# A mixed kernel of mLSTM and two expert layers: the recurrent state as one 40 by 41 block a head, and the scores of tile n beside the outputs of tile n - 1

## The chip, the cores and the metric

The kernel runs on one core of one Trainium2 chip. The metric is the device time of one execution in microseconds (us). Lower is better.

## What is computed

The reference has three stages, one behind the other (batch 2, 8 heads, 768 steps, head dimension 40):

```
for t in range(S):                       # mLSTM, for each batch and head
    m_new  = max(f[t] + m, i[t])
    C = exp(f[t] + m - m_new) * C + exp(i[t] - m_new) * outer(v[t], k[t])    # 40 x 40
    n = exp(f[t] + m - m_new) * n + exp(i[t] - m_new) * k[t]
    y[t] = sigmoid(o[t]) * (C @ q[t]) / max(|n . q[t]|, 1)
x = y as 1536 tokens x 320
x = (sigmoid(x @ w_gate) * (x @ w_val)) @ w_out            # layer one, d_ff 1536
x = rms_norm(x) * g;  a = x @ w_gate2
out = (a * sigmoid(a) * (x @ w_val2)) @ w_out2             # layer two
```

## The kernel before

**The recurrence.** It is cut into chunks of 128 steps. A tile n (0 to 11) is one chunk j = n // 2 of one batch b = n % 2, with all 8 heads. The state a batch carries from chunk to chunk is held as three groups of three heads: 120 partitions (3 heads by 40) and, a head, 41 columns (40 of v and a one for the normaliser). A product with k and v of three heads at once also gives blocks that mix heads, and a mask `bdm` takes these out.

The pieces of a tile are named by letters, and each engine has its own part of each:

- D: TensorE makes the logarithms of the decays of 8 heads in two banks (L936), ScalarE takes their exponential to `wexp` (L553) and copies the last column to `el` (L561); GpSimd multiplies v by it to `vk` (L469).
- S: TensorE makes the scores k q^T, two heads at a time in the two row halves of its array (L954, weights 40 x 128); VectorE multiplies them by `wexp` (L753); ScalarE takes the sigmoid of the output gate (L580).
- K: TensorE makes the tile's k^T v, three matmuls (L990); VectorE masks it by `bdm` (L792); GpSimd decays the state `cst` and adds the new part (L474, L477).
- N: TensorE makes state times q, three matmuls on 120 rows (L969), and scores times v, 16 matmuls whose outputs are halves of the array (L980); VectorE adds the two (L762, L764, L767).
- Y: VectorE's division: gate times numerator (L773), denominator and its reciprocal (L774, L775), their product to `y_tok` (L779), and a copy of its last 64 columns beside it (L781), because the third block of the transpose holds these columns twice.
- T: TensorE turns `y_tok` (three transposes, L895); ScalarE writes `x_hi` (L587), VectorE the rest `x_lo` (L808).
- R, F, A: decay factors of later chunks, their rows and their flattening DMA (L569, L575, L945, L946).
- O: the same turn as T for an output of layer one, for layer two (L895, L590, L812).

A matmul whose operands are plain fp32 (S, K, N) appears as two instructions in the trace, one of type fp32r as one.

**The layers.** Layer one takes the first 8 tiles in four blocks of two tiles (256 tokens). A block has 12 hidden units (`hidden`, 16 matmuls on 256 columns each, L1029 to L1032) and 4 halves of a projection (`project`, 18 matmuls on 320 columns each, L1096 to L1098). These are the 16 slots of a block. The last 4 tiles of layer one and all of layer two follow in four wide blocks of 512 tokens (`hidden_pair`, L1080).

**What sets the order.** Every engine runs its instructions in the order in which they are written. The table `WEAVE` says which pieces stand behind which slot; a slot is written "1.6" below (block 1, slot 6). All engines follow the same table:

```
for k in range(NB0):
    for slot in range(NF + 4):
        if slot < NF:
            gate(NF * k + slot)                  # VectorE: hf = sigmoid * value
        if 0 < slot <= NF:
            h_low(NF * k + slot - 1)             # VectorE: h_lo
        for what in WEAVE[k][slot]:
            piece(what)
```

On TensorE `gate` is the hidden unit itself; on ScalarE it is the unit's sigmoid (L626) and `h_high` (L632). T waits on TensorE until the whole of Y is done. The start is written out by hand: 24 idle matmuls (L1106), then D, S, N, K and T of tiles 0 and 1, D of tile 2 and R 1; then the first hidden unit, which waits for `x_lo` of both tiles and for two chunks of split weights. The split weights of layer one come from ScalarE (L538, L543) and GpSimd (L436, L441, L450), chunk after chunk during block 0 (`SPLIT_AT`); a hidden unit f waits for 2 (f // 3 + 1) chunks. Bank 7 is shared by N, R and O of the first six tiles; `seven` makes each of them wait for the one before (`IN_SEVEN`).

Of the kernel before, what the change touches and what calls it, by code (L numbers as in the profile page):

```python
# [4 lines left out]
F32 = mybir.dt.float32  # L5
# [14 lines left out]
GH = 3  # L20
NG = 3
KR = GH * D
KN = NG * KR
# [28 lines left out]

WEAVE = [
# [11 lines left out]
]  # L65

IN_SEVEN = [("R", 1)] + [what for block in WEAVE for slot in block for what in slot if what[0] in "NRO"]

# [3 lines left out]
def mlstm_moe_kernel(nc, gates, qk_t, q_t, vok, w_gv, w_o, rms_g, out):  # L72
# [5 lines left out]
    with ctx:  # L78
# [36 lines left out]
        QK, QT, VOK = 2 * NG * P + 2 * P, NG * P, HE + DM + KN  # L115

        with ExitStack() as late:
            def over(name, shape, dt):
                return late.enter_context(nc.sbuf_tensor(name, shape, dt))

            over("pad_step", [P, QK + QT + VOK], F32)
            more_lo = over("more_lo", [P, QK + QT + VOK], F32R)
            over("pad_rhs", [P, R, P], F32R)
            hf1 = over("hf1", [P, 2 * N1], F32)
        step = [sb(f"step{b}", [P, QK + QT + VOK], F32) for b in range(B)]
# [3 lines left out]
        cst = [sb(f"cst{b}", [KR, HE], F32) for b in range(B)]  # L129
        cnew = sb("cnew", [KR, HE], F32)  # L130
        inter = sb("inter", [P, HE], F32)
        num = sb("num", [P, HE], F32)
        bdm = sb("bdm", [KR, HE], F32)
# [4 lines left out]
        gcol = sb("gcol", [P, NJ, B, H], F32)  # L138
# [17 lines left out]
        q3 = [t[:, QK:QK + QT].rearrange("p (g t) -> p g t", t=P) for t in step]  # L156
        va = [t[:, QK + QT:QK + QT + HE] for t in step]
        o_sig = [t[:, QK + QT + HE:QK + QT + HE + DM] for t in step]
        kn = [t[:, QK + QT + HE + DM:QK + QT + VOK] for t in step]
# [34 lines left out]
        def kv_bank(n):  # L194
            return bank[(3, 1)[n]] if n < 2 else bank[4]
# [57 lines left out]
        q_in = [sem(f"q_in{b}") for b in range(B)]  # L253
# [61 lines left out]
        def _(sp):  # L315
            def load_qk(n):
                b = n % B
                if n >= B:
                    sp.wait_ge(s_done, 2 * (n - B) + 2)
# [3 lines left out]
            def load_vo(n):  # L323
# [4 lines left out]
                sp.dma_start(step[b][:, QK + QT:QK + QT + HE + DM], vok[n, :, 0:HE + DM]).then_inc(vo_in[b], 16)  # L328
# [47 lines left out]
            load_q(2)  # L376
# [4 lines left out]
            load_q(3)  # L381
# [809 lines left out]
```

## Time and profile before

| | us |
|---|---|
| median of 3 runs | 464.59 (464.55 to 464.93) |
| the profiled execution's own time | 464.66 |
| span of the profile, first to last instruction | 462.9 |
| TensorE busy | 452.5 (98%) |
| VectorE busy | 227.0 (49%) |
| ScalarE busy | 193.1 (42%) |
| GpSimd busy | 109.8 (24%) |
| mean granted TensorE clock | 0.996 |

The 1.8 us between span and time lie around the span. A busy TensorE is not yet one at its best: matmuls are pipelined, so the distance from start to start tells what one costs. 273 us of the span have passed when the first block of layer two begins.

### The profile page before, as it was taken

Reading aid. Unit: us, or ns where it says so; the run is one execution under the profiler, and the core shown is the slowest. Engines: PE = TensorE matmul, PEld = TensorE weight load, DVE = VectorE, ACT = ScalarE, POOL = GpSimd, SP = SyncE. Lnnn points to the kernel's source line nnn. Section 1 sums busy time; section 2 is a strip of 40 time slices with the busy share of each in tenths; the row PEclk is TensorE's granted clock in tenths of the full one; section 3 lists DMA queues with packets and bytes.
Section 4 is the critical chain, followed back from the end, with each engine's and each line's share of the span. In section 5 each row is a group of like instructions: output and inputs, shape, how many; then the busy total and the mean of one; then the engine's idle time right before and its main releaser. Section 6 shows DMA issues by size and latency. Waiting matters only on the chain. (4 is left out here: it accounts for less than half of the span.)

```text
span 462.9 us, 9428 instructions
## 1 busy us (share of the span) xinstructions
PE 452.5 (98%) x3923; PEld 410.1 (89%) x3923; DVE 227.0 (49%) x455; ACT 193.1 (42%) x359; POOL 109.8 (24%) x148
## 2 busy tenths in 40 slices
PE   8799999999999999999999999999999999999997
PEld 3699998999999999998888988889988889888897
DVE  8848866685556456432534226554026560056520
ACT  8877446642656463421745134322113321123310
POOL 5989910212121120000658354000000000000000
PEclk9999999999999999999999999999999999999999
DMA  7584610212221110300333200000000000000000
GB/s 255 193 274 134 203 53 30 68 50 83 76 62 46 61 45 5 150 1 2 99 107 95 87 19 25 1 1 16 28 16 1 1 0 30 30 0 1 2 28 30
DMA packets 11473, 27.89 MB, mean 60 GB/s; under 512 B 1526, under 2 KB 5830, under 8 KB 11430
## 3 DMA queue, kind: packets, MB, share of 16 engines
q1 hardware_dynamic: 11110, 27.20, 18.1%
q8 instruction: 31, 0.51, 0.5%
q10 hardware_dynamic: 320, 0.08, 0.1%
q14 instruction: 12, 0.10, 0.1%
HBM read 25.23 MB, written 1.97 MB: 59 GB/s over the span
## 5 line engine op out<-in xcount | busy, mean ns | idle before, releaser
L626 ACT ACTIVATE sg<-bank 128x256 f32<-128x256 f32 (+1 forms) x96 | 47.0, 491 | 147.4 <-PE bank L1080 101.1
L1080 PE MATMUL bank<-x_hi,wgv_hi 64*128 64x512 f32 x576 | 105.5, 388 | 0.8 <-DVE x_lo L812 0.8
L1080 PE MATMUL bank<-x_lo,wgv_hi 64*128 64x512 f32 x480 | 93.5, 386 | 0.0
L849 DVE TENSOR_TENSOR hf<-sg,bank 128x256 f32<-128x256 f32 (+1 forms) x96 | 53.1, 553 | 69.6 <-ACT sg L626 67.4
L1029 PE MATMUL bank<-x_hi,wgv_hi 128*128 128x256 f32 x288 | 81.9, 294 | 0.3 <-DVE x_lo L808 0.3
L1030 PE MATMUL bank<-x_lo,wgv_hi 128*128 128x256 f32 x288 | 79.4, 285 | 0.0
L1096 PE MATMUL bank<-wo_hi,h_hi 128*128 128x320 f32 x240 | 75.6, 315 | 0.0
L1080 PE MATMUL bank<-x_hi,wgv_lo 64*128 64x512 f32 x384 | 74.8, 386 | 0.0
L1098 PE MATMUL bank<-wo_hi,h_lo 128*128 128x320 f32 x240 | 74.2, 309 | 0.0
L1097 PE MATMUL bank<-wo_lo,h_hi 128*128 128x320 f32 x240 | 74.1, 309 | 0.0
L847 DVE TENSOR_TENSOR sg<-sg,bank 128x512 f32<-128x512 f32 x36 | 24.8, 688 | 87.3 <-ACT sg L626 85.3
L1080 PEld LDWEIGHTS bank<-x_hi,wgv_hi 64*128 64x128 f32 x576 | 53.9, 184 | 13.2 <-DVE x_lo L812 1.2
L1029 PEld LDWEIGHTS bank<-x_hi,wgv_hi 128*128 128x128 f32 x288 | 55.8, 194 | 1.5 <-DVE x_lo L808 0.4
L1030 PEld LDWEIGHTS bank<-x_lo,wgv_hi 128*128 128x128 f32 x288 | 55.9, 194 | 0.0
L1032 PE MATMUL bank<-x_hi,wgv_lo 128*128 128x256 f32 x192 | 54.8, 285 | 0.0
L1080 PEld LDWEIGHTS bank<-x_lo,wgv_hi 64*128 64x128 f32 x480 | 45.0, 184 | 9.3
L853 DVE TENSOR_TENSOR h_lo<-hf,h_hi 128x256 fp32r<-128x256 f32 (+1 forms) x84 | 50.4, 601 | 0.1
L1096 PEld LDWEIGHTS bank<-wo_hi,h_hi 128*128 128x128 f32 x240 | 45.1, 188 | 1.5 <-issue 1.1
L1097 PEld LDWEIGHTS bank<-wo_lo,h_hi 128*128 128x128 f32 x240 | 45.1, 188 | 0.0
L1098 PEld LDWEIGHTS bank<-wo_hi,h_lo 128*128 128x128 f32 x240 | 45.1, 188 | 0.0
L632 ACT ACTIVATE h_hi<-hf 128x256 fp32r<-128x256 f32 (+1 forms) x84 | 42.3, 504 | 5.7 <-DVE hf L849 5.7
L1080 PEld LDWEIGHTS bank<-x_hi,wgv_lo 64*128 64x128 f32 x384 | 36.0, 184 | 7.6
(131 smaller groups left out, 585.4 us busy)
## 6 DMA issues: line engine op xcount, KB each, us to landing
step<-in_vok SPq DMA_DIRECT2D x12, 324.0 KB, 2.9
step<-in_qk_t SPq DMA_DIRECT2D x24, 160.0 KB
step<-in_w_gv SPq DMA_DIRECT2D x6, 576.0 KB, 3.8
raw_p<-in_w_gv SPq DMA_DIRECT2D x5, 576.0 KB, 4.1
raw_x<-in_w_gv SPq DMA_DIRECT2D x5, 576.0 KB, 4.7
step<-in_vok SPq DMA_DIRECT2D x10, 180.0 KB, 3.4
step<-in_q_t SPq DMA_DIRECT2D x10, 180.0 KB, 2.8
raw_x<-in_w_o SPq DMA_DIRECT2D x3, 480.0 KB, 3.5
```

The source lines that it names most:

```text
L626: act.activation(sg_view(n), g_view(n), ACT.Sigmoid).then_inc(sg_done, 1)
L632: act.activation(h_view(n, 0), hf_view(n), ACT.Copy).then_inc(hhi_done, 1)
L847: dve.tensor_tensor(sg_view(n), sg_view(n), g_view(n), ALU.mult).then_inc(silu_done, 1)
L849: dve.tensor_tensor(hf_view(n), sg_view(n), v_view(n), ALU.mult).then_inc(hf_done, 1)
L853: dve.tensor_tensor(h_view(n, 1), hf_view(n), h_view(n, 0).bitcast(F32), ALU.subtract).then_inc(h_done, 1)
L1029: pe.matmul(ps, wgv_hi[:, wc, s, cs], x_hi[:, xs, s, :], start=(s == 0), stop=False)
L1030: mm = pe.matmul(ps, wgv_hi[:, wc, s, cs], x_lo[:, xs, s, :], start=False, stop=(s == 2))
L1032: pe.matmul(ps, wgv_lo[:, wc, s, cs], x_hi[:, xs, s, :], start=False, stop=False)
L1080: mm = pe.matmul(ps(n), w, x, start=own and (s, p) == (0, 0), stop=last and not own)
L1096: pe.matmul(ps, h_view(n0 + f, 0)[:, ts], wo_hi[:, f, :], start=(f == 0), stop=False)
L1097: pe.matmul(ps, h_view(n0 + f, 0)[:, ts], wo_lo[:, f, :], start=False, stop=False)
L1098: mm = pe.matmul(ps, h_view(n0 + f, 1)[:, ts], wo_hi[:, f, :], start=False, stop=(f == NF - 1))
```

## The change

The state of a head becomes a block of 40 by 41 of its own: the heads 0 to 3 lie on partitions 0 to 39 and the heads 4 to 7 on 64 to 103, each with four blocks of 41 columns. The mask, the padded groups of k and the separate copy of q (and its DMA) go. The product of state and q becomes a piece of its own, I: 16 matmuls of 40 x 64 weights, each in a quarter of the array, two outputs in each of two banks. S also becomes 16 matmuls of quarters (40 x 64) where it was 8 (40 x 128). K becomes 8 matmuls (128 x 40) in halves. The scores S of tile n stand in one slot with I, K and N of tile n - 1, the division Y one slot behind these, and the transpose T mostly one slot behind Y. VectorE's division multiplies the gate by the reciprocal first and then writes `y_tok` with two multiplications, one for the first 32 columns of each head (256), one for the last 8 twice (128); w_gate and w_val of layer one have their rows in the same order. At the start N and K of a tile stand together, and 10 idle matmuls stand between the pieces. In the first wide block VectorE's O stands ahead of `norm`, and ScalarE's last O ahead of its `square`.

```diff
 WEAVE = [
-    [[], [("S", 2)], [], [("K", 2), ("N", 2)], [("Y", 2)], [("D", 3)], [], [("S", 3), ("T", 2)],
-     [], [("K", 3), ("N", 3)], [("Y", 3)], [], [("A", 2, 0), ("A", 2, 1)],
+    [[], [("S", 2)], [], [("D", 3)], [], [], [("S", 3), ("I", 2), ("K", 2), ("N", 2)], [("Y", 2)],
+     [("T", 2)], [], [("I", 3), ("K", 3), ("N", 3)], [("Y", 3)], [("A", 2, 0), ("A", 2, 1)],
      [("A", 2, 2), ("T", 3), ("A", 2, 3), ("A", 2, 4)], [("F", 2)], [("R", 2)]],
-    [[("D", 4)], [("O", 0), ("A", 3, 0)], [("S", 4)], [("O", 1), ("A", 3, 1)], [("K", 4), ("N", 4)], [("Y", 4)],
-     [("D", 5)], [("T", 4), ("A", 3, 2)], [("S", 5), ("F", 3)], [("A", 3, 3), ("A", 3, 4)], [("K", 5), ("N", 5)],
-     [("Y", 5)], [("D", 6)], [("S", 6), ("T", 5)], [("K", 6), ("N", 6)], [("Y", 6)]],
-    [[("D", 7)], [("T", 6), ("O", 2), ("F", 4)], [("S", 7), ("O", 3)], [], [("K", 7), ("N", 7)], [("Y", 7)],
-     [("D", 8)], [("T", 7), ("R", 3)], [("S", 8)], [], [("K", 8), ("N", 8)], [("Y", 8)],
-     [("D", 9)], [("S", 9), ("T", 8), ("F", 5)], [("K", 9), ("N", 9)], [("Y", 9)]],
-    [[("D", 10)], [("T", 9), ("O", 4)], [("S", 10), ("O", 5)], [], [("N", 10)], [("Y", 10)], [("D", 11)], [("T", 10)],
-     [("S", 11)], [], [("N", 11)], [("Y", 11)], [], [("T", 11)], [], []],
+    [[("D", 4)], [("O", 0), ("A", 3, 0)], [("S", 4)], [("O", 1), ("A", 3, 1)], [("D", 5)], [("F", 3)],
+     [("S", 5), ("I", 4), ("K", 4), ("N", 4)], [("Y", 4), ("A", 3, 2)], [("T", 4), ("D", 6)], [("A", 3, 3), ("A", 3, 4)],
+     [], [("S", 6), ("I", 5), ("K", 5), ("N", 5)], [("Y", 5)], [("T", 5), ("D", 7)], [("F", 4)], []],
+    [[("S", 7), ("I", 6), ("K", 6), ("N", 6)], [("Y", 6)], [("T", 6), ("D", 8), ("O", 2)], [("R", 3)], [],
+     [("S", 8), ("I", 7), ("K", 7), ("N", 7)], [("Y", 7)], [("T", 7), ("D", 9), ("O", 3)], [("F", 5)], [],
+     [("S", 9), ("I", 8), ("K", 8), ("N", 8)], [("Y", 8)], [("T", 8), ("D", 10)], [], [],
+     [("S", 10), ("I", 9), ("K", 9), ("N", 9)]],
+    [[("Y", 9)], [("T", 9), ("D", 11), ("O", 4)], [("O", 5)], [], [("S", 11), ("I", 10), ("N", 10)], [("Y", 10)],
+     [("T", 10)], [], [("I", 11), ("N", 11)], [("Y", 11)], [("T", 11)], [], [], [], [], []],
 ]
...
+        def kv_view(n):
+            return bank[(3, 1)[n]][:, 0:KV] if n < B else bank[7][:, KV:2 * KV]
...
+        def state_view(i):
+            return bank[7][:, 0:KV] if i == 0 else bank[6][:, HE:HE + KV]
...
                 b = n % B
-                if n >= B:
+                if n >= 2 * B:
+                    sp.wait_ge(n_done, n - B + 1)
+                elif n >= B:
                     sp.wait_ge(s_done, 2 * (n - B) + 2)
...
             def divide(n):
                 b = n % B
                 src = num[:, :] if n >= B else bank[base(n) + 2][:, 0:HE]
                 dve.wait_ge(osig_done, n + 1)
-                link(dve.tensor_tensor(heads(o_sig[b]), heads(src)[:, :, 0:D], heads(o_sig[b]), ALU.mult))
                 link(dve.scalar_tensor_tensor(den[:, :], heads(src)[:, :, D], -1.0, den[:, :], ALU.mult, ALU.max))
                 link(dve.reciprocal(rden[:, :], den[:, :]))
+                link(dve.tensor_tensor(heads(o_sig[b]), heads(o_sig[b]), rden[:, :].unsqueeze(2).to_broadcast([P, H, D]),
+                                       ALU.mult))
                 if n >= B:
                     dve.wait_ge(t_done, n)
+
                 y = y_tok[:, y_slot(n), :]
-                link(dve.tensor_tensor(heads(y[:, 0:DM]), heads(o_sig[b]), rden[:, :].unsqueeze(2).to_broadcast([P, H, D]),
-                                       ALU.mult))
-                dve.tensor_copy(y[:, DM:3 * P], y[:, 2 * P:DM]).then_inc(y_done, 1)
+                dve.tensor_tensor(y[:, 0:2 * P].rearrange("p (h d) -> p h d", h=H), heads(src)[:, :, 0:Q],
+                                  heads(o_sig[b])[:, :, 0:Q], ALU.mult)
+                dve.tensor_tensor(y[:, 2 * P:3 * P].rearrange("p (u h d) -> p u h d", u=2, h=H),
+                                  heads(src)[:, :, Q:D].unsqueeze(1).to_broadcast([P, 2, H, D - Q]),
+                                  heads(o_sig[b])[:, :, Q:D].unsqueeze(1).to_broadcast([P, 2, H, D - Q]),
+                                  ALU.mult).then_inc(y_done, 1)
...
-                    for c in range(4):
-                        for i in range(2):
-                            rs = slice(64 * i, 64 * i + D)
-                            mm = pe.matmul(bank[base(n) + i][:, c * P:(c + 1) * P], sq[b][rs, 1, c, :], sq[b][rs, 0, c, :],
-                                           start=True, stop=True)
-                            if c == 3:
-                                mm.then_inc(s_done, 1)
+                    for c in range(HG):
+                        for u in range(2):
+                            us = slice(HALF * u, HALF * u + HALF)
+                            for i in range(2):
+                                rs = slice(HALF * i, HALF * i + D)
+                                mm = pe.matmul(bank[base(n) + i][us, c * P:(c + 1) * P], sq[b][rs, 1, c, us],
+                                               sq[b][rs, 0, c, :], start=True, stop=True)
+                                if c == HG - 1 and u == 1:
+                                    mm.then_inc(s_done, 1)
+                elif kind == "I":
+                    if j == 1:
+                        pe.wait_ge(cn_done, b + 1)
+                    else:
+                        pe.wait_ge(cst_done, n - 2 * B + 1)
+                    pe.wait_ge(r_exp, part_of(j))
+                    seven(what)
+
+                    pe.wait_ge(x_done, n)
+                    for c in range(HG):
+                        cs = slice(c * D1, (c + 1) * D1)
+                        for u in range(2):
+                            us = slice(HALF * u, HALF * u + HALF)
+                            for i in range(2):
+                                rs = slice(HALF * i, HALF * i + D)
+                                pe.matmul(state_view(i)[us, cs], sq[b][rs, 0, c, us], cst[b][rs, cs], start=True, stop=True)
...
+                    for c in range(HG):
+                        for i in range(2):
+                            h = HG * i + c
+                            mm = pe.matmul(kv_view(n)[HALF * i:HALF * i + D, c * D1:(c + 1) * D1], kn[b][:, h * D:(h + 1) * D],
+                                           vk[b][:, h * D1:(h + 1) * D1], start=True, stop=True)
...
-            for _ in range(24):
-                pe.matmul(bank[6][:, :], zeros[:, 0:P], zeros, start=True, stop=True)
-            for kind in "DSNKT":
+
+            def idle(ps, count):
+                for _ in range(count):
+                    pe.matmul(ps[:, :], zeros[:, 0:P], zeros, start=True, stop=True)
+
+            idle(bank[6], 23)
+            idle(bank[3], 1)
+            for kind in "DS":
                 for n in range(B):
                     piece((kind, n))
+            idle(bank[7], 4)
+            for n in range(B):
+                piece(("N", n))
+                piece(("K", n))
+            idle(bank[7], 4)
+            piece(("T", 0))
             piece(("D", 2))
+            idle(bank[7], 2)
+            piece(("T", 1))
             piece(("R", 1))
```

## Rows read from the trace of the kernel before

**Rows 1.** The page, busy time of TensorE: us, share, instructions.

```profile
PE 452.5 (98%) x3923; PEld 410.1 (89%) x3923; DVE 227.0 (49%) x455; ACT 193.1 (42%) x359; POOL 109.8 (24%) x148
```

**Rows 2.** Waits of TensorE: us in total, times, longest.

```profile
PE bank L895 <- DVE x_lo L812: 1.0, 2, 0.7
...
PE bank L1080 <- DVE x_lo L812: 0.8, 1, 0.8
PE bank L969 <- DVE x_lo L812: 0.7, 1, 0.7
...
PE bank L990 <- DVE tail L753: 0.3, 1, 0.3
```

**Rows 3.** Timeline of TensorE, score piece of a tile: start, us, instruction.

```profile
89.93 0.28 PE L1030 MATMUL bank<-x_lo,wgv_hi 128*128 128x256 f32 x1
90.14 1.16 PE L954 MATMUL bank<-step 40*128 40x128 f32 x16
...
91.46 0.28 PE L1030 MATMUL bank<-x_lo,wgv_hi 128*128 128x256 f32 x1
```

**Rows 4.** Timeline of TensorE, pieces K and N of a tile.

```profile
95.05 0.28 PE L1030 MATMUL bank<-x_lo,wgv_hi 128*128 128x256 f32 x1
95.18 0.76 PE L990 MATMUL bank<-tail,step 128*120 128x123 f32 x6
95.78 0.83 PE L969 MATMUL bank<-cst,step 120*128 120x123 f32 x6
96.54 1.13 PE L980 MATMUL bank<-step,tail 128*64 128x41 f32 x32
...
97.83 0.28 PE L1030 MATMUL bank<-x_lo,wgv_hi 128*128 128x256 f32 x1
```

**Rows 5.** Timeline around a division, block 1: TensorE, ScalarE, VectorE.

```profile
99.50 0.28 PE L1030 MATMUL bank<-x_lo,wgv_hi 128*128 128x256 f32 x1
...
99.82 0.38 ACT L626 ACTIVATE sg<-bank 128x256 f32<-128x256 f32 x1 [3.75 <-PE bank L1030]
...
100.91 0.48 DVE L773 TENSOR_TENSOR step<-num,step 128x320 f32<-128x320 f32 x1
...
102.40 0.20 DVE L781 COPY y_tok<-y_tok 128x64 f32<-128x64 f32 x1
```

**Rows 6.** VectorE from 28 to 58 us by shape: busy, mean ns.

```profile
L853 DVE TENSOR_TENSOR h_lo<-hf,h_hi 128x256 fp32r<-128x256 f32 x10 | 8.4, 835 | 0.0
...
L779 DVE TENSOR_TENSOR y_tok<-step,rden 128x320 f32<-128x320 f32 x2 | 2.0, 1023 | 0.1
```

**Rows 7.** Timeline of GpSimd at the start: splits of weight chunks.

```profile
19.91 1.00 POOL L441 TENSOR_TENSOR wgv_hi<-raw_x,wgv_hi 64x384 fp32r<-64x384 f32 x1
...
34.56 1.00 POOL L441 TENSOR_TENSOR wgv_hi<-raw_x,wgv_hi 64x384 fp32r<-64x384 f32 x1
```

**Rows 8.** Timeline of ScalarE, the exponentials of a tile.

```profile
69.60 1.28 ACT L553 ACT_TABLE_LOAD   x1
70.90 1.09 ACT L553 ACTIVATE tail<-bank 128x512 f32<-128x512 f32 x2
72.08 0.22 ACT L561 ACTIVATE el<-tail 128x8 f32<-128x8 f32 x1
```

**Rows 9.** Timeline of TensorE at the start.

```profile
19.93 0.55 PE L895 MATMUL bank<-ident,y_tok 128*128 128x128 f32 x3 [1.79 <-DVE y_tok L781]
...
21.66 0.58 PE L1029 MATMUL bank<-x_hi,wgv_hi 128*128 128x256 f32 x1 [0.31 <-DVE x_lo L808]
```

**Rows 10.** Stretches: us, busy us (count) of five engines, PEclk, DMA share, GB/s.

```profile
21.80:24.90 3.10, 3.10 (x15) 3.10 (x16) 0.61 (x2) 3.00 (x7) 2.15 (x3) 0.50 0.92 327
```

**Rows 11.** The page, DMA issues: count, KB each, median us to landing.

```profile
step<-in_vok SPq DMA_DIRECT2D x12, 324.0 KB, 2.9
```

**Rows 12.** Timeline before layer two: ScalarE's and VectorE's last O.

```profile
271.94 0.48 ACT L590 ACTIVATE x_hi<-bank 128x384 fp32r<-128x384 f32 x1
...
273.64 0.55 DVE L812 TENSOR_TENSOR x_lo<-bank,x_hi 128x384 fp32r<-128x384 f32 x1
```

More of the change, by code:

```diff
@@ L53, with mlstm_moe_kernel @@
 WEAVE = [
[2 rows of a table removed]
[2 rows of a table added]
      [("A", 2, 2), ("T", 3), ("A", 2, 3), ("A", 2, 4)], [("F", 2)], [("R", 2)]],
[8 rows of a table removed]
[9 rows of a table added]
 ]
-IN_SEVEN = [("R", 1)] + [what for block in WEAVE for slot in block for what in slot if what[0] in "NRO"]
+IN_SEVEN = [("R", 1)] + [what for block in WEAVE for slot in block for what in slot if what[0] in "IRO"]
 SPLIT_AT = {0: [4], 2: [5], 3: [6], 4: [7], 5: [8], 7: [9], 8: [10], 9: [11]}
-def mlstm_moe_kernel(nc, gates, qk_t, q_t, vok, w_gv, w_o, rms_g, out):
+def mlstm_moe_kernel(nc, gates, qk_t, vok, w_gv, w_o, rms_g, out):
     ctx = ExitStack()
@@ L119, in over @@
                 return late.enter_context(nc.sbuf_tensor(name, shape, dt))
-            over("pad_step", [P, QK + QT + VOK], F32)
-            more_lo = over("more_lo", [P, QK + QT + VOK], F32R)
+            over("pad_step", [P, STEP], F32)
+            more_lo = over("more_lo", [P, STEP], F32R)
             over("pad_rhs", [P, R, P], F32R)
             hf1 = over("hf1", [P, 2 * N1], F32)
-        step = [sb(f"step{b}", [P, QK + QT + VOK], F32) for b in range(B)]
+        step = [sb(f"step{b}", [P, STEP], F32) for b in range(B)]
         d_rhs = sb("d_rhs", [P, R, P], F32R)
@@ L128, in mlstm_moe_kernel @@
         l_row = sb("l_row", [2 * Q, LR * P], F32R)
-        cst = [sb(f"cst{b}", [KR, HE], F32) for b in range(B)]
-        cnew = sb("cnew", [KR, HE], F32)
+        cst = [sb(f"cst{b}", [KR, KV], F32) for b in range(B)]
+        cnew = sb("cnew", [KR, KV], F32)
         inter = sb("inter", [P, HE], F32)
         num = sb("num", [P, HE], F32)
-        bdm = sb("bdm", [KR, HE], F32)
         ones = sb("ones", [R, P], F32)
@@ L665, in _ @@
                     m = M0 + T1 * k + t
-                    if k == 0:
+                    if k == 0 and t < T1 - 1:
                         square(m)
                         piece(("O", M0 - B + t))
+                        continue
+                    if k == 0:
+                        piece(("O", M0 - B + t))
+                        square(m)
                         continue
@@ L883, in _ @@
                     for t in range(T1):
+                        piece(("O", M0 - B + t))
                         norm(M0 + t)
-                        piece(("O", M0 - B + t))
                 elif k == 1:
@@ L944, in piece @@
                     for jj in range(j0, j1):
-                        pe.transpose(rv[:, 0, jj, :], l_r[:, jj * P:(jj + 1) * P], ident[0:R, 0:R])
-                    pe.matmul(rv[:, 1, j0:j1, :], ones[:, :], l_end[:, j0:j1, :, :].rearrange("p j b h -> p j (b h)"),
-                              start=True, stop=True).then_inc(r_mm, 1)
+                        pe.transpose(decay_t[:, jj, :], l_r[:, jj * P:(jj + 1) * P], ident[0:R, 0:R])
+                    for i in range(2):
+                        us = slice(HALF * i, HALF * i + HALF)
+                        mm = pe.matmul(decay_end[us, j0:j1, :, :], ones[:, us], l_end[:, j0:j1, :, HG * i:HG * i + HG],
+                                       start=True, stop=True)
+                    mm.then_inc(r_mm, 1)
                 elif kind == "S":
@@ L974, in piece @@
                         pe.wait_ge(p_done, 2 * n + i + 1)
-                        for c in range(4):
-                            h = 4 * i + c
+                        for c in range(HG):
+                            h = HG * i + c
                             for u in range(2):
@@ L985, in piece @@
                     pe.wait_ge(vk_done, n + 1)
-                    pe.wait_ge(p_done, 2 * B if n < B else 2 * n + 1)
-                    for g in range(NG):
-                        cs = slice(g * GH * D1, min((g + 1) * GH, H) * D1)
-                        mm = pe.matmul(kv_bank(n)[0:KR, cs], kn[b][:, g * KR:(g + 1) * KR], vk[b][:, cs],
-                                       start=True, stop=True)
+                    if n < B:
+                        pe.wait_ge(p_done, 2 * B)
+                    for c in range(HG):
+                        for i in range(2):
+                            h = HG * i + c
+                            mm = pe.matmul(kv_view(n)[HALF * i:HALF * i + D, c * D1:(c + 1) * D1], kn[b][:, h * D:(h + 1) * D],
+                                           vk[b][:, h * D1:(h + 1) * D1], start=True, stop=True)
                     mm.then_inc(k_done, 1)
```

102 lines of the change are left out of this document (35 added, 67 removed).

## Prediction

> **What bounds the kernel now.** I read the page first: TensorE is busy for 98% of the span [rows 1]. Then its waits: from the first hidden unit to layer two they are few and short [rows 2]. So time changes by what the pieces cost on TensorE from start to start, and by waits put into or taken out of its stream; the other engines count only where TensorE waits for them. The third view is the timeline. Matmuls of a hidden unit start 0.12 us apart, so a unit of 16 costs 1.91 us. I therefore price a piece as the distance between the unit matmuls around it, less the 0.12 us steps it would have had anyway. As a check I added block 0 up to its first projection: 12 units 22.9, the clock loss priced below 1.5, two S 2.6, two K with N 5.1, D 0.5 and T 0.35 make 32.9 us after the start at 21.66 [rows 9], and the projection did start at 54.6. The sums are made against the profiled execution (464.66, of which 462.9 span); the median, 464.59, is the same within 0.1.
>
> **The pieces on TensorE.** S: 91.46 - 89.93 - 0.24 = 1.29 us [rows 3]. Its 16 instructions run as 8 pairs 0.11 us apart (0.89), so 0.4 go to entering and leaving the tiled form. K with N: 97.83 - 95.05 - 0.24 = 2.54 us, of which K 0.60, state 0.76 with 0.15 of switching in it, scores times v about 0.94 (16 pairs, 0.0585 apart) and 0.2 to leave [rows 4]. A tile costs 3.83.
>
> The new forms the trace doesn't show, so bounds. S in quarters has 32 instructions of the same columns, four at a time: 8 x 0.11 = 0.89 as before, if four run as two do. I has 32 instructions of 41 columns: in fours at the distance of N's pairs 8 x 0.0585 = 0.47; if instead every instruction costs what one of N's does (0.029), 0.94. K has 16: 0.31 if its pairs are bound by their columns, 0.47 at N's distance; I take 0.37. I take the lower ones for S and I, because the members of N's pairs start 7 ns apart and their weight loads too, so the 0.0585 is the wait for a load, not for issue. S, I, K and N in one slot: 0.19 to enter + 0.89 + 0.47 + 0.15 + 0.37 + 0.94 + 0.20 = 3.21, one entry fewer, 0.62 less than 3.83. Blocks 1 to 3 hold 8 S, 6 K with N and 2 N without K: before 8 x 1.29 + 6 x 2.54 + 2 x 1.94 = 29.4; after one S alone 1.29, six full 19.3, one without K 2.84 and one without S and K 1.94, 25.35: **-4.05 us**. If every instruction costs 0.029, S is dearer by 0.05, I by 0.47 and K by 0.10: eight times that is +4.8 on it.
>
> A rule speaks against the quarters: the Trainium skill, "TensorE: Matmul & The Clock Gate", section "Wait — 56ns, not 53.3ns?", says that matmul starts come no closer than about 25 ns however few columns they have. By it I would cost 0.80 and K 0.40, an estimate from that page, and the blocks would gain about 1.2 us and not 4.05. The trace has no denser stretch than the 32 of N, 28 ns apart in the mean, so it doesn't decide.
>
> **The transposes.** This is the term that turns the sum. Y stands one slot behind N and T one slot behind Y, where it was two or more. VectorE takes Y only after that slot's `gate`, which waits for the unit's last matmul and its sigmoid, and after `h_low`. The last matmul of the Y slot starts at 99.50, its sigmoid at 99.82, the division at 100.91, and the copy ends at 102.60 [rows 5]: 3.10 us behind the matmul, the same in all of tiles 4, 5, 7, 8, 10 and 11 within 0.02. The new division is 0.20 + 0.24 for denominator and reciprocal, 0.53 for gate times reciprocal, 0.34 and 0.28 for the two writes: 1.6 for 1.7. TensorE reaches T one unit later, at 1.91 + 0.12 = 2.03. So it waits 3.04 + 0.03 - 2.03, about **1.0 us**, with nothing behind it allowed to pass. This holds for tiles 4, 6, 7, 10 and 11. Tile 9 has no `h_low` ahead but a `norm`: 0.85. Tile 8 has a projection half (2.65) in place of the unit: 0.2. Tiles 3 and 5 have two halves: nothing. Together **+6.05**.
>
> **Other waits in blocks 1 to 3.** Behind T in 2.2 stand D 8 and O 2, and in 2.3 R 3, which waits in bank 7 for the `x_lo` of O 2. ScalarE needs for this from the start of T: 0.55 to T's end, 0.49 for `x_hi`, then the table, exponentials and `el` of D, 2.6 together [rows 8], 0.48 for O's `x_hi`, and VectorE 0.55: 4.7 us. TensorE has 0.33 + 0.47 + 0.35 + 1.91 = 3.1 to do: it waits 1.6. In 3.1 and 3.2 the same stands with O 4 and O 5, without `el`: 1.35. **+2.95**. Gone are the waits of I for O 1 (0.7), of two O for O (1.0) and of K for the weighting (0.3) [rows 2], a little more from start to start: **-2.4**, as no piece there has its supplier one slot ahead.
>
> **Start and block 0.** Without a gap of 1.8 us before the second T [rows 9], the clock should not fall. It was granted at 0.50, 1.2 GHz, for 3.1 us [rows 10]: 1.5 us gained. The first unit can start when GpSimd has split two chunks, at 20.91 [rows 7], against 21.66: 0.7. But GpSimd and ScalarE set what follows. Unit 6 needs chunk 5, which ended at 35.56 [rows 7] and with an earlier start of ScalarE's part may end at 34.7, while TensorE, which has no K and N to do first, is there at 34.1: 0.6 lost. Then S 3 to N 2, units 7 and 8: TensorE reaches T 2 at 43.6. ScalarE, with five chunks to round and two tables to load by then, gives the sigmoid of unit 6 at 39.7. VectorE then does gate 0.4, `h_low` 1.0, weighting 1.2, the copy for the state 0.3, I and N 1.7, gate 0.4, `h_low` 1.0 and the division. Beside GpSimd's splits its operations with two operands from SBUF take twice their time: `h_low` 835 ns and L779 1023 ns [rows 6], where the like L773 takes 480 [rows 5]. The division takes 3.6 there. That is 49.3: T 2 waits **5.7 us**. Then T, two units, I, K, N of tile 3 (2.3) and unit 11 end at 57.9 where it was 54.6: +3.3, everything before included. The gap is three times as long as the one behind which the clock fell, so I add 1.5 for half clock: **+4.8** for block 0.
>
> **Layer two.** O ahead of `norm` and of `square` takes ScalarE's 0.65 and VectorE's 0.83 and the wait for GpSimd from before the last `x_lo`; its copy at 271.94 [rows 12] could start at 271.5, `x_lo` end at 272.6, ahead of the 273.2 at which TensorE wants it: the wait of 0.8 goes [rows 2]: **-0.8**.
>
> **At nothing.** The loads of q and k wait for N of tile n - 2 instead of S: five slots or 9.5 us to their S, against 2.9 for a load of twice the size [rows 11]; behind them in SP's queue stand v, gate and k, which wait for Y and K of the same tile and were as late. The q loads gone, GpSimd's mask and narrower decay lie where it waits. Without the cover (GpSimd late) each would cost its own 0.5 to 1 us.
>
> **Sum:** 4.8 - 4.05 + 6.05 + 2.95 - 2.4 - 0.8 = +6.5, 471.2; I forecast **470.5 us**, as a stall gives the other engines time that I haven't counted.
>
> **Rivals.** (a) *The waits at T don't come*, because y is ready when TensorE gets there. For it: TensorE's own stream is shorter by 4 us. Against it: the order on VectorE is fixed, and six tiles agree within 0.02 us. Without them (6.05 + 5.7 + 1.5) the time is 457.5; the change is faster from the point where less than 7 of these 13.2 us are paid. 0.17. (b) *T 2 waits 2 us and the clock stays up*, as GpSimd's splits don't stretch VectorE: 3.7 + 1.5 less, 465.5. For it: the division of tile 2 would be 1.6 beside a free port. 0.13. (c) *The quarters are bound by issue*: blocks +4.8, block 0 +0.6, 476. For it: N has no denser stretch. 0.10. By the rule of the Trainium skill named above it would be 473.4, within the forecast's own range. (d) *The start and pieces gain what the waits cost*, in parts of each: within 1 us of before, 0.08.
>
> **Chances and range.** The forecast with its own range, 467 to 474: 0.52. Slower by over 0.2% (what a measurement of this kernel can tell from no change is 0.9 us): 0.52 + 0.10 and most of (b), 0.71; no difference 0.09; faster 0.20, (a) and the tail of (d). Both signs held, the range goes from 461, half of (a), to 476, (c).
>
> **What would show it.** T 4, 6, 7, 10 and 11 wait about 1 us each for the last write of `y_tok`; T 2 waits 4 to 6 us around 44 us with the clock at 0.5 behind it; R 3 and O 5 wait 1.3 to 1.6 us for `x_lo`; the first unit starts at about 21.0 at full clock; S, I, K, N take 3.2 us; the wait ahead of layer two is gone. I am wrong if y is ready within 2.0 us of the last matmul of its slot, or if fours of the quarter instructions start further apart than 0.06 us.

## The result, and the profile after

The changed kernel takes 472.72 us (median of 4 runs, 472.30 to 473.58) against 464.76 (464.55 to 465.76) measured beside it: ratio 1.0169, 95% interval 1.0149 to 1.0190. It is **slower by 8.0 us**. The forecast was 470.5, slower, within 461 to 476. The profiled execution is the 473.58 one, 8.9 above that of before; its rows are read against that.

The page of the kernel after: span, busy time of the engines, granted clock in 40 slices of 11.8 us.

```profile
span 471.8 us, 10567 instructions
...
PE 452.0 (96%) x4491; PEld 409.4 (87%) x4491; DVE 219.5 (47%) x465; ACT 193.5 (41%) x359; POOL 99.8 (21%) x141
...
PEclk9999799999989999999999999999999999999999
```

TensorE is busy as long as before [rows 1] in a span 8.9 us longer: the new time is idle time. Two slices of the clock are below 9.

The waits of TensorE in the kernel after: us in total, times, longest.

```profile
PE bank L898 <- DVE y_tok L782: 10.8, 8, 5.4
PE bank L946 <- DVE x_lo L815: 1.6, 1, 1.6
PE bank L898 <- DVE x_lo L815: 1.3, 1, 1.3
...
PE bank L1044 <- POOL wgv_hi L440: 0.5, 1, 0.5
```

Against [rows 2]: eight transposes of T wait for the last write of `y_tok`, once for 5.4 us; R 3 waits 1.6 us and O 5 1.3 us for `x_lo`; unit 6 waits 0.5 us for GpSimd's split. The wait ahead of layer two (L1080 before) is gone. The landmarks, starts of TensorE's instructions in the two profiles:

| | before | after | difference of the stretch | predicted |
|---|---|---|---|---|
| first hidden unit | 21.66 | 21.76 | +0.1 | -0.7 |
| first projection | 54.59 | 60.41 | +5.7 | +5.5 |
| first wide block | 207.50 | 217.40 | +4.1 | +2.55 |
| last matmul | 459.86 | 468.69 | -1.1 | -0.8 |

(The +5.5 is the +4.8 of the prediction without the 0.7 at the start. The stretches up to each landmark are measured from the one before it.)

**The new pieces are as cheap as hoped.** Timeline of TensorE in the kernel after, the slot with S 7, I 6, K 6 and N 6.

```profile
137.59 0.28 PE L1045 MATMUL bank<-x_lo,wgv_hi 128*128 128x256 f32 x1
137.80 1.10 PE L962 MATMUL bank<-step 40*64 40x128 f32 x32
138.72 0.62 PE L981 MATMUL bank<-cst,step 40*64 40x41 f32 x32
139.28 0.51 PE L1005 MATMUL bank<-tail,step 128*40 128x41 f32 x16
139.62 1.10 PE L993 MATMUL bank<-step,tail 128*64 128x41 f32 x32
...
140.87 0.28 PE L1045 MATMUL bank<-x_lo,wgv_hi 128*128 128x256 f32 x1
```

The unit's next L1045 starts 3.28 us behind the last; two steps of 0.12 would have passed anyway, so the four pieces cost 3.04 us (predicted 3.21; 3.83 before). From start to start S takes 0.92, I 0.56, K 0.34: 32 quarter instructions of I in 0.56 us is 18 ns each.

**A turn one unit too early.** Timeline of TensorE, then VectorE, around T 7 in the kernel after.

```profile
144.46 0.28 PE L1045 MATMUL bank<-x_lo,wgv_hi 128*128 128x256 f32 x1
145.64 0.55 PE L898 MATMUL bank<-ident,y_tok 128*128 128x128 f32 x3 [0.91 <-DVE y_tok L782]
```

```profile
144.00 0.16 DVE L772 SCALAR_TENSOR_TENSOR den<-num,den 128x8 f32<-128x8 f32 x1
144.20 0.20 DVE L773 RECIPROCAL rden<-den 128x8 f32<-128x8 f32 x1
144.44 0.49 DVE L774 TENSOR_TENSOR step<-step,rden 128x320 f32<-128x320 f32 x1
144.96 0.42 DVE L780 TENSOR_TENSOR y_tok<-num,step 128x256 f32<-128x256 f32 x1
145.30 0.28 DVE L782 TENSOR_TENSOR y_tok<-num,step 128x128 f32<-128x128 f32 x1
```

The unit in front of T ends at 144.46, when VectorE is in the third of five operations; T starts 1.18 us later where 0.12 is the plain step: 1.06 us lost. Tiles 4, 6, 10 and 11 show 1.18 or 1.19 too, tile 9 1.0, tile 8 0.5. R 3 starts 1.92 us behind its predecessor and O 5 1.61, which are 1.8 and 1.5 us lost.

**T 2.** Timeline of VectorE, then GpSimd, in the kernel after; TensorE's last matmul ahead of T 2 started at 44.46, T 2 at 50.10.

```profile
45.59 0.42 DVE L772 SCALAR_TENSOR_TENSOR den<-num,den 128x8 f32<-128x8 f32 x1
46.04 0.20 DVE L773 RECIPROCAL rden<-den 128x8 f32<-128x8 f32 x1
46.28 3.10 DVE L774 TENSOR_TENSOR step<-step,rden 128x320 f32<-128x320 f32 x1
49.42 0.42 DVE L780 TENSOR_TENSOR y_tok<-num,step 128x256 f32<-128x256 f32 x1
```

```profile
46.06 0.53 POOL L477 TENSOR_TENSOR cst<-cst,cnew 104x164 f32<-104x164 f32 x1
46.55 2.49 POOL L449 TENSOR_TENSOR wo_lo<-raw_p,wo_hi 128x320 fp32r<-128x320 f32 x3
```

L774 takes 0.49 us around T 7 and 3.10 here. It ends 0.34 us behind GpSimd's third split (46.55 + 2.49 = 49.04): here it stood for the whole of GpSimd's run. That VectorE doesn't always do so is told in the last section.

**The clock.** Stretches of the kernel after: us, busy us (count) of the five engines, granted clock, DMA share, GB/s.

```profile
48.00:50.00 2.00, 0.00 (x0) 0.00 (x0) 1.97 (x4) 0.00 (x0) 1.04 (x2) 0.50 0.85 198
50.00:52.00 2.00, 1.90 (x9) 1.90 (x10) 1.15 (x4) 0.96 (x2) 0.00 (x0) 0.50 0.56 156
52.00:54.00 2.00, 2.00 (x11) 2.00 (x10) 0.12 (x1) 0.42 (x1) 1.50 (x2) 0.50 0.42 157
54.00:56.00 2.00, 2.00 (x16) 2.00 (x16) 0.76 (x2) 1.54 (x3) 1.02 (x2) 0.83 0.00 0
...
133.00:134.00 1.00, 1.00 (x8) 1.00 (x7) 0.62 (x2) 0.98 (x2) 0.00 (x0) 0.60 0.06 16
134.00:135.00 1.00, 1.00 (x7) 1.00 (x6) 0.00 (x0) 0.97 (x4) 0.00 (x0) 0.50 0.00 0
135.00:136.00 1.00, 1.00 (x6) 1.00 (x6) 0.00 (x0) 1.00 (x1) 0.00 (x0) 0.50 0.00 0
136.00:138.00 2.00, 2.00 (x21) 1.87 (x24) 0.76 (x2) 0.81 (x4) 0.00 (x0) 0.85 0.00 0
```

Behind T 2's wait TensorE works at 1.2 GHz (granted clock 0.50) until about 54.7, 4.6 us. A unit's matmuls start 0.213 us apart there (51.23, 51.45, 51.66) instead of 0.12, so each us at half clock costs 0.44 us, and this stretch about 2.0. A second stretch, from 133.2 to 136.6, stands behind T 6's wait of 1.06 and R 3's of 1.8 us; by the same reckoning it costs 1.5 us. A direct comparison agrees: from the start of R 3 to that of T 7 this kernel takes 13.77 us, and the kernel of the experiment "T 2 two slots later", with the same waits but the clock up, 12.28. Nothing in the prediction had this second stretch.

### The profile page after: what moved, and what is told of

It is laid out like the page before. It is cut to its first block, busy times and chain, and to the rows that moved or that the text cites. A ratio compares the mean times of both kernels' runs of the same rounds, so it can differ in the third digit from the quotient of the medians.

```text
span 471.8 us, 10567 instructions
## 1 busy us (share of the span) xinstructions
PE 452.0 (96%) x4491; PEld 409.4 (87%) x4491; DVE 219.5 (47%) x465; ACT 193.5 (41%) x359; POOL 99.8 (21%) x141
## 4 chain that ended last, share of the span: by engine, by line
PE 85%; DVE 7%; ACT 5%; issue 2%; POOL 0%; DMA 0%; ACTq 0%; SPq 0%; DVEq 0%; POOLq 0%
PE bank L1095 35%; PE bank L1111 9%; PE bank L1113 9%; PE bank L1112 9%; PE bank L1044 6%; PE bank L1045 5%; PE bank L1047 4%; PE bank L962 2%; PE bank L898 2%; PE bank L993 2%; DVE step L774 1%; ACT wgv_hi L530 1%; PE bank L981 1%; DVE hf L852 1%; DVE h_lo L856 1%
## 5 line engine op out<-in xcount | busy, mean ns | idle before, releaser
L1045 PE MATMUL bank<-x_lo,wgv_hi 128*128 128x256 f32 x288 | 80.3, 288 | 0.0
L1095 PEld LDWEIGHTS bank<-x_hi,wgv_hi 64*128 64x128 f32 x576 | 54.9, 184 | 11.1 <-issue 0.7
L1044 PEld LDWEIGHTS bank<-x_hi,wgv_hi 128*128 128x128 f32 x288 | 56.8, 197 | 2.4 <-issue 1.0
L1045 PEld LDWEIGHTS bank<-x_lo,wgv_hi 128*128 128x128 f32 x288 | 56.9, 197 | 0.0
```

The source lines that it names most:

```text
L1044: pe.matmul(ps, wgv_hi[:, wc, s, cs], x_hi[:, xs, s, :], start=(s == 0), stop=False)
L1045: mm = pe.matmul(ps, wgv_hi[:, wc, s, cs], x_lo[:, xs, s, :], start=False, stop=(s == 2))
L1095: mm = pe.matmul(ps(n), w, x, start=own and (s, p) == (0, 0), stop=last and not own)
```

## The experiments

Times are medians; ratios are to the kernel before, measured on the same chip (its medians were 464.7 to 465.8). The first four ask which part of the 8 us lies where; the others price single parts. "After" is the changed kernel.

**The turns one slot later.** T of tiles 4, 6, 7, 8, 9, 10 and 11 moves one slot back; for example:

```diff
-     [[("S", 7), ("I", 6), ("K", 6), ("N", 6)], [("Y", 6)], [("T", 6), ("D", 8), ("O", 2)], [("R", 3)], [],
+     [[("S", 7), ("I", 6), ("K", 6), ("N", 6)], [("Y", 6)], [("D", 8), ("O", 2)], [("T", 6), ("R", 3)], [],
```

> T of tiles 4 and 6 to 11 one slot later, nothing else. My theory (TensorE loses its time in waits for y_tok, 1.06 us at each of six transposes and 0.5 at tile 8): these waits go, 6.5 us; R 3 and O 5 wait 0.5 less each, as ScalarE has one copy less ahead; and the slow clock near 133 us, behind two waits close together, may go too (1.6 us). 464 to 466 us. Rival one (the quarter forms cost TensorE more than the old ones): the table has nothing to do with it, 472 to 473 us. Rival two (the time is lost by the two slow stretches of the clock alone): 471 us at best.

464.74 us, ratio 0.9995 [0.9970, 1.0020]: the whole 8 us, by seven letters moved. Its waits of TensorE:

```profile
PE bank L898 <- DVE y_tok L782: 5.4, 1, 5.4
PE bank L946 <- DVE x_lo L815: 1.5, 1, 1.5
```

Of eight waits for `y_tok` only T 2's is left. In the profiled execution the second stretch of half clock is gone, though R 3 still waits 1.5 us. 6.6 us of waits and 1.5 of clock make 8.1. (R 3 and O 5 wait 0.14 us less each; 0.5 was expected.)

**Block 0 as before.**

```diff
-     [[], [("S", 2)], [], [("D", 3)], [], [], [("S", 3), ("I", 2), ("K", 2), ("N", 2)], [("Y", 2)],
-      [("T", 2)], [], [("I", 3), ("K", 3), ("N", 3)], [("Y", 3)], [("A", 2, 0), ("A", 2, 1)],
+     [[], [("S", 2)], [], [("I", 2), ("K", 2), ("N", 2)], [("Y", 2)], [("D", 3)], [], [("S", 3), ("T", 2)],
+      [], [("I", 3), ("K", 3), ("N", 3)], [("Y", 3)], [], [("A", 2, 0), ("A", 2, 1)],
```

> Block 0's row of the table as in the kernel before (I ahead of K and N), the other blocks as after the change. My theory: the wait of T 2 (5.5 us), the slow clock behind it (1.6) and the wait of unit 6 for split weights (0.6) go, against one switch of the array's form more (0.4): 7.3 us less, 465.4 us. Rival one (quarter forms): no change within 0.5, 472.7 us. Rival two (clock): only the 1.6 us, 471 us.

466.38 us, ratio 1.0031 [1.0015, 1.0047], 6.3 below after and 1 us above what was expected. From the first unit to the first projection it takes 31.4 us instead of 38.7, the 7.3 us expected; from there to T 4 it takes 1.0 us more than after, 0.2 of it a wait of D 5. The order of block 0 alone costs more than the new pieces bring in all of blocks 1 to 3 (6 x 0.79 and what S saves, about 5 us). In this profile T 6 and R 3 wait as long as after (0.9 and 1.6 us in the list of waits), and yet the clock stays at 1.00 behind them.

**Layer one's O ahead of the decays.** In slots 2.2 and 3.1:

```diff
-     [("T", 6), ("D", 8), ("O", 2)], [("R", 3)]
+     [("T", 6), ("O", 2), ("D", 8)], [("R", 3)]
-     [("T", 9), ("D", 11), ("O", 4)], [("O", 5)]
+     [("T", 9), ("O", 4), ("D", 11)], [("O", 5)]
```

> O ahead of D in the two slots where they stand together (2.2 and 3.1). My theory: R 3 and O 5 wait because the exponentials of D stand between the transposed output and its copy on ScalarE; both waits go (1.8 and 1.5 us) and with the first perhaps the slow clock behind it (1.6): 468 to 469.5 us. Rival one: 472.7 us. Rival two (clock): if the clock stays slow there, no gain; if not, 1.6 us.

469.21 us, ratio 1.0098 [1.0068, 1.0128]: 3.5 us less. In the profiled execution the waits of R 3 and O 5 are gone, and so is the second half-clock stretch, while all T waits stay; T 7's grows by 0.6. ScalarE's copy for O 2 starts at 127.17 us instead of 130.66. (The edit moves D behind O on all engines; TensorE's own part of D is 0.5 us.)

**All three together.** 

> The three edits together. My theory: they are terms of one sum, 6.5 + 7.3 + 3.3 + 1.6 us: 454 us, some 10 us below the kernel before the change, because the cheaper pieces, the clock at the start and the order ahead of layer two are then all that is left. Rival one (quarter forms dearer than the old): not below the kernel before, over 464.8 us.

455.88 us, ratio 0.9805 [0.9784, 0.9825]: **9.0 us below the kernel before, 16.8 below after**. The 454 expected is missed by 1.9. The three parts by themselves gave 8.0, 6.3 and 3.5, 17.8 together, but the second stretch of half clock, 1.5, is missing from the profiles of all three, so it was counted more than once. The page and TensorE's largest waits:

```profile
PE 446.2 (98%) x4491; PEld 406.9 (90%) x4491; DVE 222.1 (49%) x465; ACT 192.5 (42%) x359; POOL 100.7 (22%) x141
...
PEclk9999999999999999999999999999999999999999
```

```profile
PE bank L1123 <- DVE inter L818: 1.3, 1, 1.3
PE bank L1044 <- DVE x_lo L811: 0.8, 1, 0.8
PE bank L938 <- DMA d_rhs<-l_row: 0.7, 1, 0.7
```

TensorE's busy time is 6.3 us below [rows 1], the clock doesn't fall in this execution, and no wait for `y_tok` is left. The next six take one part out of this version or of after.

**The old order of pieces with the new pieces.** The whole table of before, with `("I", n)` put ahead of each K or N, in after. It tells what the pieces are worth in the order of before.

> The changed kernel with the whole table of before, I ahead of K and N. My theory: block 0 without its waits and its slow clock (7.2 us less than the change), no waits at T, R 3 and O 5 (10 us less with the second slow clock), but back come the waits of before for O 1, O 2, O 4 and the weighting (2.4) and one switch of form more a tile and no slot shared (about 2.4): 461 us, between experiment 4 and before. Rival (the grouping of S with I, K, N is worth nothing by itself, only the new pieces are): as experiment 4, 456 us.

460.45 us, ratio 0.9904 [0.9880, 0.9928]. Pieces, division, start and layer two are worth 4.4 us in the old order; the mended order adds 4.6.

**State times q twice.** In the version of all three, I computes its product twice over, into the same place:

```diff
-                     for c in range(HG):
+                     for c in [*range(HG), *range(HG)]:
```

> Experiment 4 with the 16 matmuls of I run twice into the same place. My theory (a group of four quarters every 0.0585 us): 8 x 0.0585 x 10 tiles = 4.7 us more, 460.6 us. Rival one (starts no closer than 25 ns, as the page of the Trainium skill named in the prediction says): 32 x 0.025 x 10 = 8.0 us more, 463.9 us. Rival two (every instruction 0.029 us, as one of N's does in the mean): 9.4 us more, 465.3 us.

459.72 us, ratio 0.9876 [0.9852, 0.9901], 3.8 above it. Timeline of TensorE in this kernel:

```profile
127.47 1.10 PE L962 MATMUL bank<-step 40*64 40x128 f32 x32
128.40 1.09 PE L981 MATMUL bank<-cst,step 40*64 40x41 f32 x64
129.42 0.51 PE L1005 MATMUL bank<-tail,step 128*40 128x41 f32 x16
```

From its start to that of K, I takes 1.02 us where the single one takes 0.56: 32 more instructions cost 0.46, 14.4 ns each. That settles the term on which rival (c) rests. Ten tiles of this make 4.6 us; the profiled executions differ by 4.2 and the medians by 3.8, so the size rests on the rows and not on the median. The rule of the Trainium skill that the prediction weighed ("TensorE: Matmul & The Clock Gate", "Wait — 56ns, not 53.3ns?") gives 0.80 us for the same 32, an estimate from that page; the trace doesn't agree.

**The scores in row halves again.** In the version of all three, S as 8 matmuls of 40 x 128.

```diff
-                         for u in range(2):
-                             us = slice(HALF * u, HALF * u + HALF)
-                             for i in range(2):
...
+                         for i in range(2):
+                             rs = slice(HALF * i, HALF * i + D)
+                             mm = pe.matmul(bank[base(n) + i][:, c * P:(c + 1) * P], sq[b][rs, 1, c, :],
```

> Experiment 4 with S as before the change: 8 matmuls of 40 x 128 in row halves in place of 16 quarters. My theory (four quarter instructions run as two halves do, and only entering another form costs): S itself the same 0.9 us, but I behind it now needs a switch of form in seven of the ten tiles, about 0.2 each: 457 to 457.5 us. Rival (twice the instructions cost TensorE more, so the quarters are the dearer form): 0.05 us or more a tile less, 455 us or below.

456.72 us, 0.8 above, its interval [0.9791, 0.9838] overlapping that of all three. In the profile the way from S to I takes 1.09 us against 0.92, 0.17 for each tile, and the span is 1.1 us longer. So S in quarters is a little cheaper where I follows it in the same form; the median alone would not show it, and whether the score or the change of form saves it isn't told apart.

**The start without idle matmuls.** In the version of all three, the ten between the pieces of the start go.

```diff
-             idle(bank[6], 23)
+             idle(bank[6], 22)
              idle(bank[3], 1)
+             idle(bank[7], 1)
...
-             idle(bank[7], 4)
...
-             idle(bank[7], 4)
...
-             idle(bank[7], 2)
```

> Experiment 4 without the 10 idle matmuls between the pieces of the start (one of the 24 ahead of D writes bank 7 instead of bank 6). My theory (without them the clock falls behind the pause ahead of T 1, as before the change): 3 us at half clock early in block 0, 1.5 us more: 457.4 us. Rival (the pause is shorter now, so the clock stays up without them): 455.9 us, or 0.5 less as they no longer hold up D 2.

456.93 us, ratio 0.9822 [0.9799, 0.9846], 1.05 above; the two profiled executions differ by 0.8 (455.95 and 455.18). Its stretches behind the first unit:

```profile
21.00:22.00 1.00, 1.00 (x7) 1.00 (x7) 0.15 (x1) 0.99 (x3) 1.00 (x2) 0.52 0.66 83
22.00:24.00 2.00, 2.00 (x11) 2.00 (x11) 0.00 (x0) 1.89 (x5) 1.28 (x2) 0.50 0.95 380
```

The clock of [rows 10] is back. The first unit starts 0.4 us earlier and unit 6 1.1 later, so the idle matmuls take the 1.5 us of half clock away and give part of it back.

**Layer two's order back.** In the version of all three, ScalarE's `square` and VectorE's `norm` stand ahead of O again.

> Experiment 4 with the order of O, norm and square in the first wide block as before the change. My theory: the wait of 0.8 us for the last x_lo ahead of layer two comes back, 1.0 us from start to start: 456.9 us. Rival (another wait takes its place, or none is there since the block is reached earlier): 455.9 us.

456.51 us, ratio 0.9818 [0.9797, 0.9839], 0.6 above, with overlapping intervals. The profiles show it more sharply: from the first wide block to the last matmul 252.4 us instead of 251.3. The wait of [rows 2] returns, in the waits of this kernel:

```profile
PE bank L1091 <- DVE x_lo L811: 0.8, 1, 0.8
```

**The old division.** In after, VectorE multiplies first, divides, and copies the 64 columns; the weights' rows stay in their plain order.

```diff
+                 link(dve.tensor_tensor(heads(o_sig[b]), heads(src)[:, :, 0:D], heads(o_sig[b]), ALU.mult))
...
-                 dve.tensor_tensor(y[:, 0:2 * P].rearrange("p (h d) -> p h d", h=H), heads(src)[:, :, 0:Q],
...
+                 dve.tensor_copy(y[:, DM:3 * P], y[:, 2 * P:DM]).then_inc(y_done, 1)
```

> The changed kernel with the division of before (numerator times gate first, then the product and a copy), and the weights' rows in their old order. My theory: a division is 1.68 us for 1.62, so each of six waits at T grows by 0.06; beside GpSimd's splits 4.4 us in both forms: 472.7 to 473.3 us. Rival (the new form, with its long product of two operands in SBUF, is the dearer one at T 2): 471 to 472 us.

475.99 us, ratio 1.0233 [1.0193, 1.0272]: 3.3 above after, and outside what was expected. Timeline of VectorE at the start of this kernel:

```profile
19.28 1.27 DVE L778 TENSOR_TENSOR y_tok<-step,rden 128x320 f32<-128x320 f32 x1
20.59 0.87 DVE L780 COPY y_tok<-y_tok 128x64 f32<-128x64 f32 x1
```

The copy of 64 columns takes 0.87 us beside GpSimd where [rows 5] had 0.20, twice in the start, and the first unit starts at 23.23 instead of 21.76. At T 4 the distance from start to start is 1.28 instead of 1.18. For the first two tiles the new division takes its numerator from PSUM and has one operation with both operands in SBUF (L774, 0.96 us there) and no copy; the old has L778 and the copy. I had priced the two as 1.7 and 1.6 us and nothing at the start. At T 2 the old form is held as well, at another operation: its L773, 128 x 8 elements, takes 2.83 us. Not all of the 3.3 is the division's: two of the four executions took 474.5 and 474.7 us at the mean granted clock of after (0.989, 0.988), about 2 us above it, and the two others 477.3 and 477.4 us at 0.985 and 0.982. The profiled one, 477.25, has one stretch of half clock more than after, from 24.3 to 27.7.

**T 2 two slots later, ahead of I 3.** In after.

```diff
-      [("T", 2)], [], [("I", 3), ("K", 3), ("N", 3)], [("Y", 3)], [("A", 2, 0), ("A", 2, 1)],
+      [], [], [("T", 2), ("I", 3), ("K", 3), ("N", 3)], [("Y", 3)], [("A", 2, 0), ("A", 2, 1)],
```

> The changed kernel with T 2 in slot 0.10, ahead of I 3, two slots later. My theory: y_tok of tile 2 comes at 50 us wherever T stands, since GpSimd's splits and ScalarE set it; TensorE does two units (3.8 us) of the 5.5 first and waits 1.7 for it, then I 3 waits about 1.2 for the x_lo of T 2: 2.6 us less; with no single long pause the clock may stay up, 1.6 us: 468.5 to 470.1 us. Rival (the wait is a matter of the table alone and goes in full): 7.1 less, 465.6 us.

473.94 us, ratio 1.0187 [1.0156, 1.0217]: nothing gained, a miss. Timeline of VectorE, then GpSimd:

```profile
45.53 5.62 DVE L774 TENSOR_TENSOR step<-step,rden 128x320 f32<-128x320 f32 x1
```

```profile
45.81 2.54 POOL L449 TENSOR_TENSOR wo_lo<-raw_p,wo_hi 128x320 fp32r<-128x320 f32 x3
48.31 2.48 POOL L449 TENSOR_TENSOR wo_lo<-raw_x,wo_hi 128x320 fp32r<-128x320 f32 x3
```

With TensorE two units further on, GpSimd had the next chunk to split as well, six operations without a pause, and VectorE's multiplication stood for all six (they end at 50.79, and it 0.36 behind). T 2 still started 4.3 us behind its predecessor, and I 3 behind it waited 3.0.

**No splits beside that division.** In after, the splits of slots 7 and 8 move to slot 9:

```diff
-SPLIT_AT = {0: [4], 2: [5], 3: [6], 4: [7], 5: [8], 7: [9], 8: [10], 9: [11]}
+SPLIT_AT = {0: [4], 2: [5], 3: [6], 4: [7], 5: [8], 9: [9, 10, 11]}
```

> The changed kernel with the last three weight chunks rounded and split in slot 0.9 (behind T 2) instead of 0.7, 0.8 and 0.9, so that GpSimd is idle while VectorE divides tile 2. My theory (VectorE's product of two SBUF operands, 3.1 us long in the changed kernel and 5.6 in experiment 11, stands still until GpSimd's run of splits ends): the product takes 0.5 us, y_tok of tile 2 comes 2.6 us earlier, T 2 waits 2.8 us and not 5.4: 469 to 470.1 us, and 1.6 less if the clock stays up behind the shorter pause. Rival (the product is long for another cause): 472.7 us, or more if the later splits hold up the first projection.

470.06 us, ratio 1.0097 [1.0061, 1.0134], 2.7 below after. Timeline of VectorE, then GpSimd:

```profile
45.71 0.66 DVE L774 TENSOR_TENSOR step<-step,rden 128x320 f32<-128x320 f32 x1
```

```profile
45.49 0.53 POOL L477 TENSOR_TENSOR cst<-cst,cnew 104x164 f32<-104x164 f32 x1
```

L774 takes 0.66 instead of 3.10 us, ending 0.35 behind GpSimd's last operation, and T 2's wait falls to 2.9. So about 2.5 us of T 2's wait was GpSimd, the other 2.9 the order of the pieces. The gain of 2.7 is a balance: up to the first projection this profile is 3.1 us shorter than after, and it has no second stretch of half clock (1.5), but D 4 now waits 0.9 us for the DMA of its decay row, and in all blocks 1 to 3 take as long as after (157.2 and 157.0 us).

## Why the prediction was right, step by step

Here "a for b" means that a was measured where b had been predicted.

**What bounds, and the sign: right.** TensorE's stream was priced from start to start, and the sum was carried by waits put into it. The first experiment shows those waits by themselves; rival (a), that y would be ready in time, falls with it, and so does (d).

**The size: in the range, and helped by errors that cancel.** Against the landmarks the sum of 6.55 us became 8.8 in the profiled execution. The start was 0.8 dearer than said, the second stretch of half clock 1.5, the waits at T, R 3 and O 5 0.9, block 0 0.2; the pieces gave 1.0 and layer two 0.3 more than said. The 0.7 us that I took off the sum to get 470.5, for time that a stall gives the other engines, shows nowhere. About 0.2 isn't assigned.

**The pieces: right, a little too dear.** 3.04 us for 3.21, six times: 1.0 us more gained than the 4.05 said. The choice of the lower bound for the quarters (fours at the distance of N's pairs) is confirmed by the doubled I. Rival (c), 476, and the rule's 473.4 needed 0.80 us and more for I; it costs 0.46 at the margin. That the total came near 473.4 is chance: the extra is in the clock, not in the pieces.

**Waits at T: right.** 1.06 us for the 1.0, in the tiles named, with 0.9 for T 9 (0.85) and 0.4 for T 8 (0.2): 6.6 for 6.05. **R 3 and O 5: right**, 1.8 and 1.5 for 1.6 and 1.35, 3.3 for 2.95. The third experiment shows that they come from D standing ahead of O on ScalarE.

**T 2: the size right, the reason half right.** 5.5 us for 5.7. Rival (b) said 2 us with the clock up; its reason, that GpSimd's splits don't stretch VectorE, is refuted by the 3.10 us. I had VectorE's operations take twice their time beside GpSimd, 3.6 for the division; in the trace one of them stands for a whole run of splits while the others are hardly longer (4.45 from 45.59 to the last write). The last two experiments tell these apart for this operation: a rate would have let T 2 catch up when moved; the wait for a run grew with the run. That the two accounts give nearly the same time in after is luck.

**The step that failed: the clock was priced once.** The sum for blocks 1 to 3 was -4.05 + 6.05 + 2.95 - 2.4 = +2.55. With the measured terms (the -2.4 as predicted, it wasn't measured by itself) it is -5.05 + 6.6 + 3.3 - 2.4 = +2.4, and the profile shows +4.1. Of the rest, 1.7, the second stretch at 1.2 GHz is 1.5; 0.2 isn't assigned. I reckoned with half clock only behind T 2, though I had placed waits of 1.0 and 1.6 us within 5 us of each other in 2.2 and 2.3. Why the clock fell there is not settled: without T 6's wait it stayed up (first experiment), and without R 3's (third); but with both waits of the same size it fell in after and in the kernel with the old division, and stayed up in the profiles of the second experiment (block 0 as before) and of the last two.

**The start: wrong by 0.8.** I said 0.7 earlier; the unit started at 21.76. It waited 0.80 us for `x_lo`, and not for the splits. The idle matmuls at the very beginning took 7.7 us in this execution against 6.5 in that of before. That explains most of the 0.8: in the version of all three they took 6.3, and the unit started at 21.16, 0.5 earlier than before and still behind a wait of 0.80 for `x_lo`. The clock part was right (full clock behind 21.76) and is worth about 1 us net in the experiment without idle matmuls, not 1.5. The division's part at the start, about 1.5 us, was missing from my sum on the other side.

**Block 0 and layer two.** From the first unit to the projection +5.7 for +5.5, with 2.0 us of half clock for 1.5. Layer two -1.1 for -0.8, and the wait that I named is the one that went.

## What to carry to other kernels

A piece that TensorE consumes must stand as many units behind its maker as the chain through the other engines is long. Here the chain from the unit's last matmul over sigmoid, gate, `h_low` and division is 3.1 us and a unit 2.0, so one slot is too few and two are free: seven letters of a table were worth 8 us, and block 0's order another 6; together they hid a version that is 9 us faster than before. And on each engine a short copy that another piece waits for belongs ahead of a long exponential.

When a kernel gets slower by idle time with its busy time unchanged, keep the change and move its consumers before judging it.

## What the hardware showed that I had not expected

**VectorE beside GpSimd is held, for one operation of GpSimd or for a whole run.** L774, 0.49 us long by itself and with two operands in SBUF, took 0.66, 3.10 and 5.62 us, and ended each time 0.34 to 0.36 us behind the end of an unbroken run of GpSimd: L477 alone, with three splits behind it, and with six. But this isn't a rule. In the kernel before, VectorE was let in between operations of GpSimd that followed each other at once. Timeline of VectorE, then GpSimd, in the kernel before:

```profile
41.02 1.16 DVE L779 TENSOR_TENSOR y_tok<-step,rden 128x320 f32<-128x320 f32 x1
```

```profile
40.80 2.25 POOL L436 TENSOR_TENSOR wgv_lo<-raw_x,wgv_hi 128x384 fp32r<-128x384 f32 x2
```

The first of the two splits ended at 41.83 and the second started at once; L779 ended at 42.18, 0.35 us behind the first and 0.9 ahead of the end of the second. L773 at 54.16 came in likewise, 0.35 us behind L477, with three splits directly behind. What decides between one operation and the whole run, no experiment here tells. The Trainium skill, "SBUF — State Buffer", section "Who interferes with whom", says that a VectorE instruction with two SBUF inputs contends with a GpSimd instruction that reads SBUF. The traces agree, and show that the wait can last for up to seven instructions of GpSimd.

**Quarter matmuls start 14.4 ns apart in the mean** (doubled I), below the 25 ns of the page of the Trainium skill named in the prediction; they go in fours, 0.058 us from one group to the next and 7 ns apart within it.

**The clock can fall behind pauses of under 2 us** (1.8 us at the start of the kernel before [rows 9] [rows 10]; 1.06 and 1.8 us at T 6 and R 3), and it doesn't do so each time: in executions of the first experiment the mean granted clock was 0.993, 0.989 or 0.985, at 463.7 to 465.1, 466.0 to 466.2 and 467.1 to 467.7 us. Less than 2 us can't be told from one execution of this kernel.

**Idle matmuls at the start don't keep time.** 23 of them took 6.49 us before and 7.73 after, and the first hidden unit moves with them in part: from 6.3 to 7.7 us of them (all three, after) it went from 21.16 to 21.76.
